# A four-stage attention and MoE kernel: weight sums on other engines, an earlier load, and a shifted operand

## What is computed

```python
scores = scale * x @ state.T;   a  = softmax(scores);  xread = a @ state
scores2 = scale * state @ x.T;  a2 = softmax(scores2); sread = a2 @ x
x = concat([xread, sread])              # 4352 x 512
h = maximum(x @ w_in, 0);  y = h * h @ w_out        # 512 -> 2048 -> 512
a, b = y @ w1, y @ w2                               # 512 -> 1024 each
out = ((a * b) @ w3) @ w_out2                       # 1024 -> 1024 -> 512
```

## Time and profile before

| | |
|---|---|
| median of 3 runs | 1301.54 us (1298.03 to 1304.68) |
| the profiled execution | 1298.76 us; its span 1297.2 us |
| mean granted clock of TensorE | 0.989 of full |
| PE busy | 1248.2 us, 96% |
| DVE busy | 835.7 us, 64% |
| ACT busy | 476.6 us, 37% |
| POOL busy | 147.3 us, 11%, 164 instructions |

### The profile page before, as it was taken

The page is one execution under the profiler, slowest core; times in us unless marked ns, Lnnn a source line. Parts: engine busy times, 40 slices in busy tenths (PEclk is TensorE's granted clock), DMA queues, the critical chain, the costliest instruction groups (busy, mean ns, idle before and its releaser), DMA issues.

```text
span 1297.2 us, 19431 instructions
## 1 busy us (share of the span) xinstructions
PE 1248.2 (96%) x7177; PEld 1083.0 (83%) x7177; DVE 835.7 (64%) x1397; ACT 476.6 (37%) x904; POOL 147.3 (11%) x164
## 2 busy tenths in 40 slices
PE   8979999999999989899999989999999999999998
PEld 6657888877877768778888989999999999999998
DVE  6666877678686786876554465666566665757541
ACT  6565554534445344454444231212122121212111
POOL 1000000044262442610000000000000000000000
PEclk9988999999999999999999999999999999999999
DMA  8986431143433434331123770101010101010210
GB/s 297 363 295 210 137 129 55 64 155 135 141 129 122 145 120 130 130 126 59 42 98 122 252 266 11 66 1 65 0 65 0 65 0 65 3 61 0 82 50 33
DMA packets 63092, 139.10 MB, mean 107 GB/s; under 512 B 5184, under 2 KB 6208, under 8 KB 63040
## 3 DMA queue, kind: packets, MB, share of 16 engines
q1 hardware_dynamic: 51680, 96.49, 22.2%
q0 software_dynamic: 11360, 41.95, 9.2%
HBM read 84.93 MB, written 53.48 MB: 107 GB/s over the span
## 4 chain that ended last, share of the span: by engine, by line
PE 80%; DVE 11%; DMA 3%; ACT 3%; issue 2%; SPq 0%; DVEq 0%; ACTq 0%; POOL 0%; POOLq 0%
PE ps_y L674 39%; PE ps_h L674 21%; PE ps_t L674 18%; DVE t L1201 3%; ACT v_hi L964 2%; DVE GA L1201 1%; DVE s L1201 1%; DVE v_lo L1201 1%; DVE aT_lo L1201 1%; DMA g_scratch<-g_extra 1%; DMA wp_scratch<-stage 1%; DVE x_lo L1201 1%; DMA raw<-y_scratch 1%; DMA g_scratch<-stage 1%; PE ps_h L733 1%
## 5 line engine op out<-in xcount | busy, mean ns | idle before, releaser
L964 ACT CAST v_hi<-t 128x512 fp32r<-128x512 f32 (+1 forms) x216 | 128.9, 597 | 538.4 <-DVE t L1201 533.8
L674 PE MATMUL ps_y<-v_hi,X_hi 128*128 128x512 f32 (+1 forms) x576 | 223.3, 388 | 25.4 <-DVE v_lo L1201 23.1
L1201 DVE TENSOR_TENSOR v_lo<-t,v_hi 128x512 fp32r<-128x512 f32 (+1 forms) x216 | 150.3, 696 | 147.9 <-ACT v_hi L964 147.9
L674 PE MATMUL ps_y<-v_lo,X_hi 128*128 128x512 f32 (+1 forms) x576 | 219.9, 382 | 0.0
L674 PE MATMUL ps_y<-v_hi,X_lo 128*128 128x512 f32 (+1 forms) x576 | 219.2, 381 | 0.0
L1201 DVE TENSOR_TENSOR t<-t 128x256 f32<-128x256 f32 (+1 forms) x272 | 160.9, 611 | 83.9 <-ACT t L1050 81.5
L674 PEld LDWEIGHTS ps_y<-v_hi,X_hi 128*128 128x128 f32 x576 | 109.7, 190 | 52.9 <-DVE v_lo L1201 31.1
L674 PEld LDWEIGHTS ps_y<-v_hi,X_lo 128*128 128x128 f32 x576 | 109.9, 191 | 21.0
L1050 ACT ACTIVATE t<-ps_h 128x512 f32<-128x512 f32 (+1 forms) x144 | 82.3, 572 | 119.9 <-PE ps_h L674 119.4
L674 PEld LDWEIGHTS ps_y<-v_lo,X_hi 128*128 128x128 f32 x576 | 109.9, 191 | 19.1
L1201 DVE TENSOR_TENSOR t<-t,ps_t 128x256 f32<-128x256 f32 (+1 forms) x132 | 72.6, 550 | 48.1 <-PE ps_t L674 34.3
(11 more groups left out here) (232 smaller groups left out, 2885.2 us busy)
## 6 DMA issues: line engine op xcount, KB each, us to landing
raw<-g_scratch SPq DMA_DIRECT2D x64, 256.0 KB
s_scratch<-top POOLq DMA_DIRECT2D x32, 512.0 KB, 3.8
raw<-in_moe_w_in SPq DMA_DIRECT2D x32, 256.0 KB
raw<-in_x_T SPq DMA_DIRECT2D x32, 256.0 KB
raw<-in_x_tok SPq DMA_DIRECT2D x32, 256.0 KB
y_scratch<-stage POOLq DMA_DIRECT2D x8, 1024.0 KB, 5.5
raw<-y_scratch SPq DMA_DIRECT2D x8, 1024.0 KB, 5.3
out<-stage POOLq DMA_DIRECT2D x8, 1024.0 KB, 4.6
```

The source lines that it names most:

```text
L674: mm = nc.tensor.matmul(dst, w, m, start=first and n == 0, stop=last and n == 2)
L964: return nc.scalar.copy(dst, src)
L1201: return nc.vector.tensor_tensor(dst, a, b, op)
```

## The change

The weight sums go to ScalarE and VectorE, into the chunks of blocks 1 to 4 (`S_part`, called from `h_chunk` between relu or square and `v_hi` or `v_lo`): in chunks 2, 3, 5, 7, 8, 10, 11 and 13 ScalarE casts a block and VectorE subtracts; in chunks 4, 6, 9 and 12 VectorE makes a sum. There are two buffers for the parts. SyncE loads the four blocks of weights behind the fourth piece of a block; GpSimd only stores, hi and lo separately, ahead of the block's y. SyncE loads the first y block and four pieces of w' before all sets of weights; the sums of y move to slot 8, the token sets to slots 9 to 13. `SHIFT` is 88.

```diff
+    SHIFT = 88
...
-    SHIFT = 80
...
-        top_f = nc.alloc_sbuf_tensor_at("top_f", [P, N_SETS, C], F32, offset=TOP_AT)
+        top_f = nc.alloc_sbuf_tensor_at("top_f", [P, 5, C], F32, offset=TOP_AT)
...
-                      .rearrange("p (j k n) -> p j k n", j=N_SETS, k=2)[:, :, :, 0:HT] for t in (X_hi, X_lo))
+                      .rearrange("p (j k n) -> p j k n", j=N_SETS, k=2) for t in (X_hi, X_lo))
...
+        parts = [(top[:, 5], top[:, 6]), (E_lo[:, 6], E_lo[:, 7])]
+        A11, A12, A21, A22, S3 = (top_f[:, k] for k in range(5))
+        work = {2: (A11, 0), 3: (A21, 7), 5: (S3, 2), 7: (A21, 3), 8: (A22, 5), 10: (A11, 1), 11: (A12, 4),
+                13: (A12, 6)}
+        total = {4: (S3, A11, A21, ALU.subtract), 6: (A21, A21, A22, ALU.add), 9: (A11, A21, A11, ALU.subtract),
+                 12: (A12, A12, A11, ALU.subtract)}
+        order_S = [j for _, j in work.values()]
+
+        def A_block(half, kk, row, col):
+
             c = 2 * col + kk
-            return (moe2_w1, moe2_w2)[row][c * P:(c + 1) * P, half * C:(half + 1) * C]
+            return (moe2_w1, moe2_w2)[row].rearrange("k (s n) -> s k n", n=C)[half][c * P:(c + 1) * P, :]
...
-        S_step = sem("S_step")
-        S_stored = sem("S_stored")
+        S_total = sem("S_total")
+        S_rounded = sem("S_rounded")
+        S_split = sem("S_split")
+        S_stored = [sem("S_stored0"), sem("S_stored1")]
...
-        set_slots = {10: [0], 11: [1, 2], 12: [3, 4], 13: [5, 6]}
+        set_slots = {9: [0], 10: [1], 11: [2, 3], 12: [4], 13: [5, 6]}
...
-            def tile(b, slot_lists, r0, i=0):
+            def tile(b, slot_lists, r0, i=0, kk=None):
                 for n, piece in enumerate(flat(slot_lists)):
                     load_piece(r0 + n, piece, b, i, 2 * PT)
+                    if kk is not None and n == 3:
+                        sp.wait_ge(S_split, i * 2 * KINDS + kk * KINDS + 1)
+                        for dst, row, col in ((A11, 0, 0), (A12, 0, 1), (A21, 1, 0), (A22, 1, 1)):
+                            sp.dma_start(dst, A_block(i, kk, row, col)).then_inc(A_loaded, 16)
...
-            with sp.Fori(0, (NB - 2) // 2) as i:
-                tile(2 * i + 1, tile_slots, R_1, i)
-                tile(2 * i + 2, tile_slots, R_1 + PT, i)
+            with sp.Fori(0, (NB - 4) // 2) as i:
+                tile(2 * i + 1, tile_slots, R_1, i, 0)
+                tile(2 * i + 2, tile_slots, R_1 + PT, i, 1)
+            for b in range(NB - 3, NB - 1):
+                tile(b, tile_slots, R_1 + (b - 1) * PT)
...
-            sp.wait_ge(S_stored, 16 * 4 * KINDS)
+            sp.wait_ge(piece_split, N_RING)
+            sp.wait_ge(y_stored, 16)
+            load_y(y_main[0])
+            sp.wait_ge(wp_stored, 16 * 2)
+            for k in range(4):
+                load_wp(k)
+            for stored_part in S_stored:
+                sp.wait_ge(stored_part, 16 * 4 * KINDS)
             load_S(0, 1, range(N_SETS))
             sp.wait_ge(h_full, KF * NB)
...
             load_S(1, 0, range(N_SETS))
-            sp.wait_ge(piece_split, N_RING)
-            sp.wait_ge(y_stored, 16)
-            load_y(y_main[0])
-            sp.wait_ge(wp_stored, 16 * 2)
-            for k in range(4):
-                load_wp(k)
...
+            nc.gpsimd.memset(A11[:, 0:1], 0.0).then_inc(S_split, 1)
...
-            def S_weights(g):
-                A11, A12, A21, A22, S3 = (top_f[:, k] for k in range(5))
-                n = g * (4 + 2 * KINDS)
-                stores = g * KINDS
-                for dst, row, col in ((A11, 0, 0), (A12, 0, 1), (A21, 1, 0), (A22, 1, 1)):
-                    pool.dma_start(dst, A_block(g, row, col)).then_inc(A_loaded, 16)
-                pool.wait_ge(A_loaded, 16 * 4 * (g + 1))
...
-                def split(src, j):
-                    nonlocal n, stores
-                    wait_for(pool, S_stored, 16 * stores)
-                    wait_for(pool, S_step, n)
-                    nc.gpsimd.tensor_copy(top[:, 5], src).then_inc(S_step, 1)
-                    n += 1
-                    total(top[:, 6], src, top[:, 5].bitcast(F32), ALU.subtract)
-                    pool.wait_ge(S_step, n)
-                    pool.dma_start(s_dram[g, j].rearrange("k p n -> p k n"), top[:, 5:7].bitcast(F32)).then_inc(S_stored, 16)
-                    stores += 1
...
-                split(A11, 0)
-                split(A21, 7)
...
+            def store_S(i, kk):
+                for n, j in enumerate(order_S):
+                    pool.wait_ge(S_split, i * 2 * KINDS + kk * KINDS + n + 2)
+                    dst = s_dram.rearrange("(h k) j s p n -> h k j s p n", k=2)[i][kk, j]
+                    for part in range(2):
+                        pool.dma_start(dst[part], parts[n % 2][part].bitcast(F32)).then_inc(S_stored[n % 2], 16)
 
             store_y(0, S)
-            for g in range(4):
-                store_y(g + 1, S)
-                S_weights(g)
-            for t in range(5, NB):
+            with pool.Fori(0, (NB - 4) // 2) as i:
+                for kk in range(2):
+                    store_S(i, kk)
+                    store_y(2 * i + kk + 1, S)
+            for t in range(NB - 3, NB):
                 store_y(t, S)
             store_y(SR, NT)
...
+            def S_part(f, i, kk):
+                if f in work:
+                    n = order_S.index(work[f][1])
+                    if n == 0:
+                        act.wait_ge(A_loaded, i * 2 * 64 + (kk + 1) * 64)
+                    if n > 1:
+                        act.wait_ge(S_stored[n % 2], i * 32 * KINDS + (kk * KINDS // 2 + n // 2) * 32)
+                    if f > 4:
+                        act.wait_ge(S_total, i * 8 + kk * 4 + (f > 4) + (f > 6) + (f > 9) + (f > 12))
+                    copy(parts[n % 2][0], work[f][0]).then_inc(S_rounded, 1)
+                if f == 15:
+                    for stored_part in S_stored:
+                        act.wait_ge(stored_part, i * 32 * KINDS + (kk + 1) * 16 * KINDS)
+
+            def h_chunk(t, n, f, group=None):
                 act.wait_ge(h_full, KF * t + f + 1)
                 wait_for(act, sq_done, KF * t + f - 1)
                 nc.scalar.activation(t1[:, f % 2, 0:n], ps_h[:, f % 2, 0:n], ACT.Relu).then_inc(relu_done, 1)
+                if group is not None:
+                    S_part(f, *group)
                 wait_for(act, y_full, KF * t + f - 3)
                 act.wait_ge(sq_done, KF * t + f + 1)
...
+            def S_part(f, i, kk):
+                if f == 2:
+                    dve.wait_ge(A_loaded, i * 2 * 64 + (kk + 1) * 64)
+                if f in work:
+                    n = order_S.index(work[f][1])
+                    dve.wait_ge(S_rounded, i * 2 * KINDS + kk * KINDS + n + 1)
+                    tt(parts[n % 2][1], work[f][0], parts[n % 2][0].bitcast(F32), ALU.subtract).then_inc(S_split, 1)
+                if f in total:
+                    dst, a, b, op = total[f]
+                    tt(dst, a, b, op).then_inc(S_total, 1)
+
+            def h_chunk(t, n, f, group=None):
                 dve.wait_ge(relu_done, KF * t + f + 1)
                 relu = t1[:, f % 2, 0:n]
                 tt(t2[:, f % 2, 0:n], relu, relu, ALU.mult).then_inc(sq_done, 1)
+                if group is not None:
+                    S_part(f, *group)
                 minus(v_lo[:, f % 4, 0:n], t2[:, f % 2, 0:n], v_hi[:, f % 4, 0:n], sq_hi,
...
-                if f == 9:
+                if f == 8:
                     T_sums(0)
```

More of the change, by code:

```diff
@@ L191, in build_program @@
                 v_rows + [raw_r[:, k] for k in range(3)]]
-        def A_block(g, row, col):
-            half, kk = g // 2, g % 2
+        parts = [(top[:, 5], top[:, 6]), (E_lo[:, 6], E_lo[:, 7])]
[6 more added lines that the diff above has]
+        def A_block(half, kk, row, col):
             c = 2 * col + kk
-            return (moe2_w1, moe2_w2)[row][c * P:(c + 1) * P, half * C:(half + 1) * C]
+            return (moe2_w1, moe2_w2)[row].rearrange("k (s n) -> s k n", n=C)[half][c * P:(c + 1) * P, :]
         st_zero = sem("st_zero")
@@ L607, in store_y @@
                 pool.dma_start(y_main[t] if n == S else y_rest, stage[:, :, 0:n]).then_inc(y_stored, 16)
-            def S_weights(g):
-                A11, A12, A21, A22, S3 = (top_f[:, k] for k in range(5))
-                n = g * (4 + 2 * KINDS)
-                stores = g * KINDS
-                for dst, row, col in ((A11, 0, 0), (A12, 0, 1), (A21, 1, 0), (A22, 1, 1)):
-                    pool.dma_start(dst, A_block(g, row, col)).then_inc(A_loaded, 16)
-                pool.wait_ge(A_loaded, 16 * 4 * (g + 1))
-                def total(dst, a, b, op):
-                    nonlocal n
-                    wait_for(pool, S_step, n)
-                    nc.gpsimd.tensor_tensor(dst, a, b, op).then_inc(S_step, 1)
-                    n += 1
-                def split(src, j):
-                    nonlocal n, stores
-                    wait_for(pool, S_stored, 16 * stores)
```

(20 more changed lines are left out.)

1 line of the change is left out of this document (removed).

## The result

The changed kernel took 1270.89 us (median of 4 runs, 1270.14 to 1271.18) against 1300.84 us before (median of 4, 1298.03 to 1304.68): ratio 0.9767, 95% interval 0.9741 to 0.9793. The forecast of 1265 was 5.9 us low, inside its range. The profiled execution took 1271.0 us, its span 1269.4.

A forecast was written before the change was run, and what follows sets the result against it. TensorE, busy 96% of the span, was taken as the bound, so only its waits or slow matmuls could yield: 1298.8 - 30.6 (weight sums) - 3.6 (early y load) + 0 (352 bytes) = 1264.6, given as 1265 us; range 1251 to 1279.

The forecast's parts named there:

- The weight sums: Blocks 2 to 5: sums leave GpSimd, whose operations hold VectorE; added work costs 0; gain 30.6 us, bounds 14.6 and 30.6.
- Rival B: Blocks 1 to 4: VectorE becomes the bound in the softmax chunks, some 4 us a block, 1281 us; chance 12%.
- the hole of 0.74 us: VectorE's wait for ScalarE's v_hi cast before v_lo; a moved operation of 0.69 us was to nearly fill it.
- block 0: First-stage block with VectorE busy 56.2 of 72.0 us, more than the 54.6 to come, and PE busy 71.9.
- The stores and the raw loads: Twice as many weight stores on GpSimd, raw weight loads moved to SyncE's ring: covered, the loads' cost 0.
- y first: Block of state tokens: early y load removes two PE waits of 1.7 us; gain 3.6 us, bounds 0 and 8.
- third wait: Block of state tokens: PE's 3.1 us wait for ScalarE's copy of P1, behind the last w' casts; claimed to stay.
- The clock's dip: After PE's 3.1 us wait: granted clock 0.78 for 5 us, near 1.1 us lost, left in the forecast.
- 352 bytes: Second stage's 256-column matmuls: new start of the token sets, moving operand, priced at 0, bounds 6.6 us either way.
- Rival C: Second stage: matmul pitch moves, back to 120.0 ns 1271.6 us, as far the other way 1258.4; chance 14%.
- Rival E: Second stage: new start makes moving-operand reads cost more; 11.8 ns a matmul eats the gain, 1297 or 1573 us; 3%.

The follow-up runs named there:

- the experiment outside it: Version at 320 bytes with the weights' casts, subtractions and sums behind v_hi and v_lo, out of VectorE's wait for the v_hi cast: 1264.85 us, ratio 0.9726.

## Why the prediction was right, and where it was off

**The weight sums** were forecast at -30.6 us, with that as the best case, and the blocks that they leave show -31.7: the text took 72.05 us for an undisturbed block, and they take 71.8. The mechanism is as read: GpSimd's operations hold VectorE's two-input ones, and PE waits for `v_lo` where that runs past the slack. One thing the text read too smoothly: it says that the 2.44 us of the square agree with a lock for the whole instruction, but 1.30 and 0.69 us make 1.99 at most. That the square is held agrees; why for that long stays open. Rival B (VectorE as the bound, +16 us) didn't come about. Against it the text had two reasons, the hole of 0.74 us and block 0. The hole is filled as foreseen, but the experiment outside it shows that it wasn't needed: "The cover is thus the wait itself" was wrong, and with it the 4 us a block without the hole (measured: 0). What covers the work is, by the timeline, the distance of two chunks between `h` and `y`; no run shortened that distance. Block 0, the other reason, is in line with it.

**The stores and the raw loads** cost nothing, as forecast: GpSimd's issues lengthen no instruction of VectorE (the square is 0.69 us on the mean of block 3: 16 in 11.0 us).

**y first** was forecast at -3.6. Alone it gives -3.8, the two waits of 1.7 us gone and the third as it was: right in mechanism and size. In the changed kernel the block of state tokens shows only -2.9, as its third wait is 4.7 us there. The text held that this wait "stays", and in order and cause it does: in the nine other traces with the new order of loads and w' in its slots it is 2.9 to 3.5 us, and their w' load lands 3.9 to 4.9 us after its issue. In this one execution the load took 6.1. But for the start of the token sets this kernel is the one at 320 bytes, where it took 4.8, so it looks like scatter of a load; with one trace of the changed kernel that isn't shown, and what the load met is open.

The clock's dip behind the wait, which the text left in the sum at 1.1 us, scatters as well. The kernel at 448 bytes was traced twice, with waits of 2.9 and 3.2 us. In the first execution TensorE ran at the lower level (0.50 of full, 1.2 in place of 2.4 GHz) for part of the stretch from 725 us, in the second not at all, and the block took 53.0 and 50.6 us:

```profile
725.00:730.00 5.00, 3.34 (x16) 3.37 (x17) 3.42 (x7) 1.17 (x3) 0.00 (x0) 0.60 1.04 392
```

```profile
725.00:730.00 5.00, 4.07 (x34) 4.10 (x35) 4.45 (x9) 0.94 (x3) 0.00 (x0) 1.00 1.00 381
```

So the length of this block in one trace is good to about 2.5 us, and the 50.8 us at 320 bytes (732.90 less 682.10 between y stores, no dip) are 5.8 less than before in part by luck.

**352 bytes** was priced at 0 with 6.6 us either way, and cost 6.9 us of second stage in the trace and 6.1 between the timed kernels. This is the term that was mis-sized. On the spans the change was forecast at -34.2 us and brought -27.8: +6.9 from this term, +0.7 from y, -1.1 from the sums, -0.1 elsewhere. So it is more than the whole miss. The reasoning "halfway between 117.7 and 120.0" was a guess between two points; the start at 96 past a multiple is slow, like 0. Rival C (14% for a move of the pitch by its full size either way, 1271.6 for the slow side) is what happened, and its time is right within a microsecond. The Trainium skill's gap, from which 109.2 ns can be estimated for 256 columns and which names no address (TensorE: Matmul & The Clock Gate, "Wait — 56ns, not 53.3ns?"), agrees with neither value here, and by it this term would be 0; the measured 117.8 and 120.0 decide.

The miss of 5.9 us against 1265 holds a second part, the base of the sum: it counts from the profiled execution before, 1298.76, 2.1 us under the median before of 1300.84. In medians the change brought 29.9 us, 4.3 fewer than the terms add up to.

**Rival E** (slower than before, by more than 11.8 ns a matmul) had the right place and the right sign, at a fifth of the size it needed.

## What to carry to other kernels

Look for the second engine that an instruction got slower beside, in the groups by form of two like stretches: an engine that is "only 11% busy" cost 31 us here through the instructions of another. A move onto an engine that is busier on paper can lower its busy time. When a change bundles a layout shift with real work, price the shift by running it alone: 32 bytes gave away 6 of the 36 us that the rest of this change brings.

## What the runs showed of the hardware that was not expected

- The pace of matmuls in this three-pass format depends on how the operands lie to each other: with the token sets 64 bytes past a multiple of 128 and all other operands of TensorE at one, the second stage's 256-column matmuls start 117.8 ns apart on the mean, with the sets 0 or 96 past one 119.9 and 120.1; moving everything by 64 bytes changes nothing. For the 512-column ones of the first stage it is the reverse, 227.1 ns at 0 and 229.6 at 64.
- These means hide a pattern. At 352 bytes the distances between pairs of matmuls in the second stage go from 115.8 to 125.0 ns, by the buffers that their weights lie in; at 320 bytes from 117.5 to 118.9.
- The 512-column matmuls of the second stage, whose own operands didn't move, take 229.7 ns with the sets before them at 320 bytes and 226.7 at 192 or 448. At 320 bytes it is the first of the twelve that lose: by their place in the chunk the first seven have 224 to 241 ns on the mean of some 50 chunks, the last five the 226.7 that all have at 448.
- A one-input copy on GpSimd lengthens a square on VectorE too (1.09 us beside it), if less than a two-input operation (2.44 us); on the mean of two-input operations of that size 0.98 against 1.67 us.
- The granted clock's dip behind PE's wait is not tied to that wait's length alone: on the mean of 5 us it fell to 0.79 behind 4.7 us in the changed kernel and to 0.50, the lower of its two levels, behind 3.1 in the early y load alone (760 to 765 us), and stayed at 1.00 behind 3.4 us at 320 bytes, in whose trace the stretch reads:

```profile
720.00:725.00 5.00, 2.92 (x25) 2.71 (x24) 1.98 (x5) 2.03 (x4) 0.00 (x0) 1.00 0.99 345
725.00:730.00 5.00, 3.70 (x31) 3.73 (x32) 4.65 (x10) 1.12 (x3) 0.00 (x0) 1.00 1.05 399
```

  while the kernel before fell to 0.78 behind 3.1 us.
